# Attention of a three-stage kernel: turns in another order, mask and sums interleaved, weight transfers from ScalarE, mix's first key blocks around the last apply

## The chip, the cores and the metric

The kernel runs on one core of one Trainium2 chip. The metric is the device time of one execution in microseconds (us); lower is better. Engines are called by their names in the profile: PE is TensorE (PEld its weight loads), DVE is VectorE, ACT is ScalarE, POOL is GpSimd, SP is SyncE.

## The reference

Three stages follow each other: local and global attention, a gated channel mix, and a layer with eight experts of which each token takes one. The change lies in the first stage and in the first lines of the second.

```python
# attention: B=4, H=8 heads, 512 local and 32 global positions, head size 64
s_g  = scale * q_g @ concat(k_g, k_l).T              # global queries see all keys
out_g = softmax(s_g) @ concat(v_g, v_l)
s_ll = where(abs(i - j) <= 32, scale * q_l @ k_l.T, -1e9)
s_l  = concat(scale * q_l @ k_g.T, s_ll)             # local: a band, and the global keys
out_l = softmax(s_l) @ concat(v_g, v_l)              # softmax: exp(s - max) / (sum + 1e-9)
x = concat(out_g, out_l) as rows of 512, 2176 tokens in all
# mix
xk = mu_k * x + (1 - mu_k) * x_prev;  xr likewise with mu_r
x2 = sigmoid(xr @ w_r) * (relu(xk @ w_k) ** 2 @ w_v)
# experts: out = p[e] * (relu(x2 @ w1[e]) @ w2[e]), e chosen by token from its logits
```

## The kernel before

All is written by hand: each engine has its own program, the order on an engine is the order in the code, and semaphores tie the engines together.

Attention is cut into 40 units. A batch has ten (`UNITS`), in two quads (four heads each) of five: four local units of 128 queries by 160 keys for four heads, and one global unit (the 32 global queries against all 544 keys). A unit passes through these tasks:

- PE `scores` (L601 local, 16 matmuls; L615 global, 24) writes `ps_s`, which has two buffers.
- DVE `mask_scores` (L929, one instruction and the reading of its accumulator for each head; L933 for a global unit) writes `neg` and the negated maxima. `neg` has one buffer, so the mask of unit t starts after the exponentials of t-1.
- ACT `exponentials` (L1343, one for each head, with the row sums).
- POOL `copy_edges` (L456) gathers the columns of the global keys of four heads into `edge`, and POOL `spread_sums` (L466, L468) widens the inverted sums to `rb`. DVE `invert_sums` makes these (L942 adds 1e-9, L947 inverts).
- PE `turn` transposes: half a is two heads' probabilities (L630) and `rb` (L633), half b is the two other heads (L638) and `edge` (L640). `ps_t` has one buffer of two banks. ACT `copy_turned` (L1353) copies half a, DVE `copy_turned` (L955) half b, to `probT`.
- PE `apply` multiplies `probT` with the values (L668 with the global ones, L674 with the local ones; L686, L689, L692 in a global unit). It waits for both halves before its first matmul.
- DVE `write_x` (L966, L969) multiplies with the turned inverted sums into `xT`.

In step t PE does scores(t), apply(t-2), turn(t-1); DVE does invert(t-1), mask(t), write_x(t-2), copy(t-1); ACT does exponentials(t), copy(t-1). PE, DVE and ACT hold batches 1 and later in a loop; POOL is written out.

Between the units POOL prepares the mix's weights: 20 chunks of 128x512 arrive in two raw buffers (`w_raw`) by transfers that POOL issues itself (L433), POOL rounds a chunk (L437, `round_chunk`) and subtracts (L441, `rest_of_chunk`), then it issues the load of the chunk after next. Four such parts go to three steps, so the work ends with unit 29. In the last batch ACT and DVE also form the inputs of the mix's first group (`first_inputs`), with `w_raw`'s first half as scratch (`first_raw`); ACT therefore waits for all 20 chunks there. SP loads keys, queries and values (L349 to L360), each quad's for the next batch once its global unit has been scored or applied.

The mix takes four tiles of 128 tokens as a group. For each group PE forms eight blocks f of keys, each of 12 matmuls of 512 columns (L723 to L725: high by high, high by low, low by high), in two banks of PSUM in turn. Block f waits for the square of block f-2, which ACT (L1428) and DVE (L1063) make. Both begin the mix only when all of `xT` is written.

## Time and profile before

| | |
|---|---|
| median of 3 runs | 701.54 us (699.85 to 701.92) |
| the profiled execution, its own time | 700.96 us |
| its span | 699.3 us |
| busy over the span | PE 91%, DVE 52%, ACT 40%, POOL 26% |
| PE warms up (30 transposes) until | 7.1 us |
| first apply of attention starts | 13.45 us |
| PE busy from 150 to 300 us | 147.95 us |
| first matmul of the mix starts | 134.28 us |
| granted TensorE clock, mean | 0.966 (1.00 in every window up to 300 us) |

The span is the time between the first and the last instruction of the profiled execution; 1.7 us of that execution's time lie outside it. Times within the trace count from the span's start. A busy share over the whole span mixes the three stages. For this change the stretch from 7 to 140 us counts, and there the idle time of PE, with what ended it.

### The profile page before, as it was taken

What the parts mean: (1) busy time and instruction counts of PE and PEld (TensorE: products, weight loads), DVE (VectorE), ACT (ScalarE), POOL (GpSimd) and SP (SyncE); (2) the same over time, 40 slices, a digit from 0 to 9 for tenths busy, and PEclk for the clock granted to TensorE, in tenths of its full rate; (3) what the DMA queues carried; (4) which work ended last, traced back from release to release, by engine and by line L of the source; (5) the groups of instructions that cost most, each with busy time, mean ns of one, the idle gap of its engine ahead of it and who ended that gap; (6) DMA issues with size and microseconds to landing.
All of it is one profiled execution on the core that took longest, in us unless ns stands there. A gap on an engine that the chain in (4) does not pass through costs nothing.

```text
span 699.3 us, 15184 instructions
## 1 busy us (share of the span) xinstructions
PE 637.5 (91%) x4666; PEld 527.5 (75%) x4667; DVE 366.6 (52%) x920; ACT 281.6 (40%) x615; POOL 185.2 (26%) x263
## 2 busy tenths in 40 slices
PE   7899999899999999999999703999999999999994
PEld 6787777777887787789788502887888888888883
DVE  3677778594445626445434295649253353353531
ACT  4666678444313422332321140547243252262521
POOL 5676762200000000000000064235515215124140
PEclk9999999999999999999999855999999999999997
DMA  9878871000100010010010283658526135145000
GB/s 326 314 250 280 279 256 61 2 0 1 46 15 1 19 43 0 0 45 16 1 46 1 79 312 119 207 171 304 205 81 217 60 95 215 45 134 182 10 26 3
DMA packets 29204, 78.09 MB, mean 112 GB/s; under 512 B 4330, under 2 KB 7146, under 8 KB 29168
## 3 DMA queue, kind: packets, MB, share of 16 engines
q1 hardware_dynamic: 24368, 63.47, 26.1%
q0 software_dynamic: 4800, 14.16, 5.8%
q8 instruction: 19, 0.31, 0.2%
q14 instruction: 17, 0.14, 0.1%
HBM read 69.49 MB, written 9.70 MB: 113 GB/s over the span
## 4 chain that ended last, share of the span: by engine, by line
PE 81%; DVE 7%; ACT 5%; issue 4%; DMA 1%; POOL 0%; DVEq 0%; ACTq 0%; POOLq 0%
PE banks L723 22%; PE banks L725 21%; PE banks L724 21%; ACT prob L1343 3%; PE banks L869 3%; PE banks L742 2%; PE banks L668 1%; DMA xg<-x_rows,rows_in 1%; PE banks L844 1%; PE banks L630 1%; PE banks L615 1%; ACT probT L1353 1%; PE banks L674 1%; PE banks L734 1%; PE banks L686 1%
## 5 line engine op out<-in xcount | busy, mean ns | idle before, releaser
L518 POOL TENSOR_TENSOR we_lo<-we_raw,we_hi 128x1024 f32 (+1 forms) x18 | 50.4, 2822 | 319.8 <-ACT we_hi L1462 319.8
L1316 DVE TENSOR_SCALAR hid<-banks 128x512 f32<-128x512 f32 x40 | 27.7, 692 | 94.2 <-PE banks L725 92.8
L1343 ACT ACTIVATE prob<-neg,negmax 128x160 f32<-128x160 f32 (+1 forms) x136 | 59.2, 437 | 38.6 <-DVE negmax L929 27.4
L1462 ACT ACTIVATE we_hi<-we_raw 128x1024 f32 (+1 forms) x64 | 63.8, 1051 | 12.8 <-issue 8.1
L723 PE MATMUL banks<-we_hi,hid_hi 128*128 x160 | 66.8, 418 | 1.4 <-DVE hid_lo L1321 1.4
L723 PE MATMUL banks<-we_hi,xg_hi 128*128 x160 | 65.8, 411 | 1.7 <-DVE xg_lo L1287 1.7
L724 PE MATMUL banks<-we_lo,xg_hi 128*128 x160 | 63.8, 399 | 0.0
L725 PE MATMUL banks<-we_hi,xg_lo 128*128 x160 | 63.7, 398 | 0.0
L725 PE MATMUL banks<-we_hi,hid_lo 128*128 x160 | 63.1, 395 | 0.0
L724 PE MATMUL banks<-we_lo,hid_hi 128*128 x160 | 63.1, 394 | 0.0
L723 PE MATMUL banks<-mix_hi,wm_hi 128*128 128x512 f32 (+2 forms) x160 | 58.6, 366 | 0.5 <-DVE k_raw L1063 0.3
L725 PE MATMUL banks<-mix_hi,wm_lo 128*128 128x512 f32 (+2 forms) x160 | 57.2, 358 | 0.0
L724 PE MATMUL banks<-mix_lo,wm_hi 128*128 128x512 f32 (+2 forms) x160 | 57.1, 357 | 0.0
L1291 DVE TENSOR_TENSOR we_lo<-we_raw,we_hi 128x1024 f32 (+1 forms) x46 | 56.2, 1263 | 0.0
L723 PE MATMUL banks<-wm_hi,k_hi 128*128 128x512 f32 x136 | 54.0, 397 | 1.3 <-issue 1.3
L725 PE MATMUL banks<-wm_hi,k_lo 128*128 128x512 f32 x136 | 53.2, 391 | 0.0
L724 PE MATMUL banks<-wm_lo,k_hi 128*128 128x512 f32 x136 | 53.0, 390 | 0.0
L1495 ACT ACTIVATE hid_hi<-banks 128x512 fp32r<-128x512 f32 x40 | 23.9, 598 | 71.1 <-PE banks L869 71.1
L1428 ACT COPY k_sum<-banks 128x512 f32<-128x512 f32 (+2 forms) x40 | 20.9, 522 | 78.6 <-PE banks L725 78.5
L572 POOL DMA_INDIRECT out_rows<-y,rows_out x20 | 20.6, 1032 | 97.7 <-ACT y L1510 90.7
L1063 DVE SCALAR_TENSOR_TENSOR k_raw<-banks,k_sum 128x512 f32<-128x512 f32 (+2 forms) x40 | 24.4, 611 | 40.9 <-ACT k_sum L1428 40.9
L1321 DVE TENSOR_TENSOR hid_lo<-banks,hid_hi 128x512 fp32r<-128x512 f32 x40 | 27.6, 690 | 34.2 <-ACT hid_hi L1495 34.2
(215 smaller groups left out, 1400.6 us busy)
## 6 DMA issues: line engine op xcount, KB each, us to landing
we_raw<-in_w_e SPq DMA_DIRECT2D x64, 512.0 KB, 4.4
qk<-in_qk_t SPq DMA_DIRECT2D x32, 448.0 KB, 6.1
vw<-in_v_t SPq DMA_DIRECT2D x32, 256.0 KB, 4.5
w_raw<-in_w_mix POOLq DMA_DIRECT2D x20, 256.0 KB, 4.5
x_rows<-x SPq DMA_DIRECT2D x17, 256.0 KB, 2.0
vz<-in_v_z SPq DMA_DIRECT2D x8, 128.0 KB, 2.9
vx<-in_v_x SPq DMA_DIRECT2D x8, 96.0 KB, 5.1
qg<-in_qg_t SPq DMA_DIRECT2D x8, 64.0 KB, 6.8
```

Source lines behind the costliest of these rows:

```text
L518: return pool.tensor_tensor(we_lo[:, buf, 2 * j:2 * j + 2, :].rearrange("p x a b -> p x (a b)"), we_raw[:, j, :].unsqueeze(1), we_hi[:, bu ...
L723: pe.matmul(dst, left[0], right[0], start=first, stop=False)
L724: pe.matmul(dst, left[0], right[1], start=False, stop=False)
L725: return pe.matmul(dst, left[1], right[0], start=False, stop=last)
L869: mm = pe.transpose(ps_ht[:, h, P * c:P * (c + 1)], hid[:, D * h + P * c:D * h + P * (c + 1)], ident[:])
L1063: dve.scalar_tensor_tensor(raw, ps_k[:, f % 2, 0:w], 0.0, k_sum[:, f % 2, 0:w], ALU.max, ALU.mult).then_inc(k_squared, 1)
L1291: dve.tensor_tensor(we_lo[:, buf, 2 * j:2 * j + 2, :].rearrange("p x a b -> p x (a b)"), we_raw[:, j, :].unsqueeze(1), we_hi[:, buf, 2 * j ...
L1316: dve.tensor_scalar(hid[:, D * h:D * (h + 1)], ps_h[:, h, :], 0.0, None, ALU.max).then_inc(hid_ready, 1)
L1321: dve.tensor_tensor(hid_lo[:, D * h:D * (h + 1)], ps_ht[:, h, :], hid_hi[:, D * h:D * (h + 1)].bitcast(F32), ALU.subtract).then_inc(hid_lo ...
L1343: act.activation(prob[:, t % 2, c], neg[:, c], ACT.Exp, scale=-1.0, bias=negmax[:, t % 2, k:k + 1], accum_out=rsum[:, t % 2, k:k + 1]).the ...
L1462: act.activation(we_hi[:, buf, 2 * j:2 * j + 2, :].rearrange("p x a b -> p x (a b)"), we_raw[:, j, :].unsqueeze(1), ACT.Copy).then_inc(we_ ...
L1495: act.activation(hid_hi[:, D * h:D * (h + 1)], ps_ht[:, h, :], ACT.Copy).then_inc(hid_hi_ready, 1)
```

## The change

- **Turns.** `turn` does half b first (two heads, then `edge`), then half a: two heads, and `rb` as the last. ACT's exponentials and POOL's `spread_sums` wait for half a of the turn two units back, where they waited for half b. `edge` has one buffer instead of two, so `copy_edges(t)` waits for half b of turn t-1.
- **Apply.** It waits for half b alone at first, does the four matmuls with the global values and pair 1, waits for half a, then does pair 0. A global unit does its chunks 2, 3, 4 first, then 0 and 1.
- **Mask and sums.** In a local unit the mask's first head comes first, then the addition to the sums (`guard_sums`), the second head, the inversion (`invert_sums`), and the other two heads.
- **Weights.** ACT issues the 20 transfers: two at its start, then one after each `copy_turned` of an even step, behind a wait for POOL's subtraction. POOL rounds a chunk in an even step and subtracts it in the odd one, so the work ends with step 39. `first_raw` is a tile of its own, and ACT's wait for all chunks falls away. ACT's program is written out for all batches.
- **Mix.** Block 0 of group 0 is computed between the last turn and the last apply, behind a wait for all weight chunks; block 1 right after the last apply.

```diff
-        edge = sb("edge", [P, 2, HEADS * SG], to=att)
+        edge = sb("edge", [P, HEADS * SG], to=att)
...
-        first_raw = w_raw[:, 0, :]
+        first_raw = sb("first_raw", [P, GT * P], to=att)
...
-                if n + 2 < MIX_CHUNKS:
-                    pool.wait_ge(wm_lo_ready, n + 1)
-                    load_chunk(n + 2)
...
-                if n >= 2:
-                    pool.wait_ge(turned_b, n - 1)
+                if n >= 1:
+                    pool.wait_ge(turned_b, n)
                 by_head = prob[:, t % 2, :].rearrange("p (k c) -> p k c", k=HEADS)
-                pool.tensor_copy(edge[:, t % 2, :].rearrange("p (k c) -> p k c", k=HEADS),
-                                 by_head[:, :, HALO:KW]).then_inc(edged, 1)
+                pool.tensor_copy(edge[:].rearrange("p (k c) -> p k c", k=HEADS), by_head[:, :, HALO:KW]).then_inc(edged, 1)
...
-                    for part in range(4 * n // 3, 4 * (n + 1) // 3):
-                        if part >= 2 * MIX_CHUNKS:
-                            break
-                        if part % 2:
-                            rest_of_chunk(part // 2)
+                    n, low = divmod(UNITS * b + t, 2)
+                    if n < MIX_CHUNKS:
+                        if low:
+                            rest_of_chunk(n)
                         else:
-                            round_chunk(part // 2)
+                            round_chunk(n)
...
-                for k in range(2):
-                    c = KW * k if j is not None else P * k
-                    pe.transpose(ps_t[:, 0, P * k:P * (k + 1)], pr[:, c:c + P], ident[:])
-                pe.wait_ge(spread, n + 1)
-                for k in range(2 if j is not None else 1):
-                    mm = pe.transpose(ps_t[:, 0, P * (2 + k):P * (3 + k)], rb[:, t % 2, P * k:P * (k + 1)], ident[:])
-                mm.then_inc(turned_a, 1)
                 if j is not None:
                     for k in range(2):
                         c = KW * (2 + k)
                         pe.transpose(ps_t[:, 1, P * k:P * (k + 1)], pr[:, c:c + P], ident[:])
                     pe.wait_ge(edged, local_steps(b, t) + 1)
-                    mm = pe.transpose(ps_t[:, 1, 2 * P:3 * P], edge[:, t % 2, :], ident[:])
+                    mm = pe.transpose(ps_t[:, 1, 2 * P:3 * P], edge[:], ident[:])
                 else:
                     pe.transpose(ps_t[:, 1, 0:P], pr[:, 2 * P:3 * P], ident[:])
                     pe.transpose(ps_t[0:P - WIN, 1, P:2 * P], pr[:, 3 * P:SL - WIN], ident[:])
                     mm = pe.transpose(ps_t[0:WIN + SG, 1, 2 * P:3 * P], pr[:, SL - WIN:SL + SG], ident[:])
                 mm.then_inc(turned_b, 1)
+                for k in range(2):
+                    c = KW * k if j is not None else P * k
+                    pe.transpose(ps_t[:, 0, P * k:P * (k + 1)], pr[:, c:c + P], ident[:])
+                pe.wait_ge(spread, n + 1)
+                for k in range(2 if j is not None else 1):
+                    mm = pe.transpose(ps_t[:, 0, P * (2 + k):P * (3 + k)], rb[:, t % 2, P * k:P * (k + 1)], ident[:])
+                mm.then_inc(turned_a, 1)
...
-                pe.wait_ge(probT_a, n + 1)
...
                     for pair in range(2):
                         for h in range(2):
                             pe.matmul(o[DH * h:DH * (h + 1), P * pair:P * (pair + 1)], vz[i][:, 2 * pair + h, :],
-                                      pt(HEADS), start=True, stop=False)
+                                      pt(HEADS), start=(pair == 0), stop=False)
+                    for pair in (1, 0):
+                        if pair == 0:
+                            pe.wait_ge(probT_a, n + 1)
                         for blk in range(2):
                             for h in range(2):
                                 k = 2 * pair + h
                                 v0 = HEADS * DH * blk + DH * k
                                 mm = pe.matmul(o[DH * h:DH * (h + 1), P * pair + QB * blk:P * pair + QB * (blk + 1)],
-                                               vw[i][:, j, v0:v0 + DH], pt(k, QB * blk, QB), start=False, stop=(blk == 1))
+                                               vw[i][:, j, v0:v0 + DH], pt(k, QB * blk, QB), start=False, stop=(pair == 0 and blk == 1))
...
+                    for cs in ((2, 3, 4), (0, 1)):
+                        if cs[0] == 0:
+                            pe.wait_ge(probT_a, n + 1)
...
-            apply(B - 1, UNITS - 2)
-            turn(B - 1, UNITS - 1)
-            apply(B - 1, UNITS - 1)
...
+            def keys_part(g, tiles, f):
+                half, col = divmod(P * f, D)
+                for c in range(DC):
+                    mm = three_pass(ps_k[:, f % 2, 0:P * tiles], [a[:, HALVES * c + half, col:col + P] for a in wm],
+                                    [a[0][:, c, 0:P * tiles] for a in (mix_hi, mix_lo)], c == 0, c == DC - 1)
+                mm.then_inc(k_summed, 1)
+            apply(B - 1, UNITS - 2)
+            turn(B - 1, UNITS - 1)
+            pe.wait_ge(masked, heads_done(B - 1, UNITS - 1))
+            pe.wait_ge(mix_lo_ready, DC + 2)
+            pe.wait_ge(wm_lo_ready, MIX_CHUNKS)
+            keys_part(0, GT, 0)
+            apply(B - 1, UNITS - 1)
+            keys_part(0, GT, 1)
...
-                for f in range(FC):
+                for f in range(2 if first_group(g) else 0, FC):
...
+                        if last and k == 0:
+                            guard_sums(*last)
+                        if last and k == 1:
+                            invert_sums(*last)
...
-                if behind(b, t, 1):
-                    invert_sums(*behind(b, t, 1))
-                mask_scores(b, t)
+                last = behind(b, t, 1)
+                if last and unit(t)[1] is None:
+                    guard_sums(*last)
+                    invert_sums(*last)
+                mask_scores(b, t, last)
...
+            guard_sums(B - 1, UNITS - 1)
...
-                    act.wait_ge(turned_b, UNITS * b + t - 1)
+                    act.wait_ge(turned_a, UNITS * b + t - 1)
...
-                        act.wait_ge(wm_lo_ready, MIX_CHUNKS)
...
+            def load_chunk(n):
+                act.dma_start(w_raw[:, n % 2, :], w_mix[P * n:P * (n + 1), :]).then_inc(wm_raw_loaded[n % 2], 16)
...
+                n = (UNITS * b + t) // 2
+                if t % 2 == 0 and n >= 1 and n + 1 < MIX_CHUNKS:
+                    act.wait_ge(wm_lo_ready, n)
+                    load_chunk(n + 1)
+            for n in range(2):
+                load_chunk(n)
+            for b in range(B):
                 for t in range(UNITS):
                     step(b, t)
-            for t in range(UNITS):
-                step(B - 1, t)
-                first_inputs(t)
+                    if b == B - 1:
+                        first_inputs(t)
```

Three places show the new order. First PE in one local step of the first batch (apply of unit 1, turn of unit 2), before:

```order
L668 MATMUL banks<-probT,vz 64x128 [waits quad0_v1_loaded,probT_b,probT_a]
L668 MATMUL banks<-probT,vz 64x128
L674 MATMUL banks<-probT,vw 64x64 x4
L668 MATMUL banks<-probT,vz 64x128 x2
L674 MATMUL banks<-probT,vw 64x64 x4
L630 MATMUL banks<-ident,prob 128x128 [waits probT_b,probT_a,exped]
L630 MATMUL banks<-ident,prob 128x128
L633 MATMUL banks<-ident,rb 128x128 [waits spread]
L633 MATMUL banks<-ident,rb 128x128
L638 MATMUL banks<-ident,prob 128x128 x2
L640 MATMUL banks<-ident,edge 128x128 [waits edged]
```

and now (L657 and L666 are apply, L620 to L634 turn):

```order
L657 MATMUL banks<-probT,vz 64x128 [waits quad0_v1_loaded,probT_b]
L657 MATMUL banks<-probT,vz 64x128 x3
L666 MATMUL banks<-probT,vw 64x64 x4
L666 MATMUL banks<-probT,vw 64x64 [waits probT_a]
L666 MATMUL banks<-probT,vw 64x64 x3
L620 MATMUL banks<-ident,prob 128x128 [waits probT_b,probT_a,exped]
L620 MATMUL banks<-ident,prob 128x128
L622 MATMUL banks<-ident,edge 128x128 [waits edged]
L630 MATMUL banks<-ident,prob 128x128 x2
L634 MATMUL banks<-ident,rb 128x128 [waits spread]
L634 MATMUL banks<-ident,rb 128x128
```

The wait for `probT_a` moved from the first matmul of apply to the ninth, and the transposes of `rb` from the third and fourth place of the turn to the last.

Second, DVE in one local step, before (L942 and L947 are the sums of the unit before, L929 the mask with the reading of its accumulator, L969 write_x):

```order
L942 TENSOR_TENSOR rsum<-rsum,eps 128x4 [waits exped]
L947 RECIPROCAL rinv<-rsum 128x4 [waits spread,summed]
L929 ISA neg,negmax<-banks,mask 128x160 [waits scored,exped]
L929 ISA negmax 128x1
L929 ISA neg,negmax<-banks,mask 128x160
L929 ISA negmax 128x1
L929 ISA neg,negmax<-banks,mask 128x160
L929 ISA negmax 128x1
L929 ISA neg,negmax<-banks,mask 128x160
L929 ISA negmax 128x1
L969 TENSOR_TENSOR xT<-banks,probT 128x2x128 [waits applied]
L955 COPY probT<-banks 128x384 [waits applied,turned_b]
```

and now (L951 and L959 are the sums, L932 the mask):

```order
L932 ISA neg,negmax<-banks,mask 128x160 [waits scored,exped]
L932 ISA negmax 128x1
L951 TENSOR_TENSOR rsum<-rsum,eps 128x4 [waits exped]
L932 ISA neg,negmax<-banks,mask 128x160
L932 ISA negmax 128x1
L959 RECIPROCAL rinv<-rsum 128x4 [waits spread,summed]
L932 ISA neg,negmax<-banks,mask 128x160
L932 ISA negmax 128x1
L932 ISA neg,negmax<-banks,mask 128x160
L932 ISA negmax 128x1
L981 TENSOR_TENSOR xT<-banks,probT 128x2x128 [waits applied]
L967 COPY probT<-banks 128x384 [waits applied,turned_b]
```

The mask's first head no longer stands behind the sums; the inversion stands behind two heads of the mask.

Third, ACT at the end of steps 1 and 2, before:

```order
L1353 COPY probT<-banks 128x512 [waits turned_a]
L1343 ACTIVATE prob,rsum<-neg,negmax 128x160 [waits masked,turned_b]
L1343 ACTIVATE prob,rsum<-neg,negmax 128x160 [waits masked] x3
L1353 COPY probT<-banks 128x512 [waits turned_a]
L1343 ACTIVATE prob,rsum<-neg,negmax 128x160 [waits masked,turned_b]
```

and now (L1358 is an exponential, L1368 the copy, L1388 a weight transfer):

```order
L1368 COPY probT<-banks 128x512 [waits turned_a]
L1358 ACTIVATE prob,rsum<-neg,negmax 128x160 [waits masked,turned_a]
L1358 ACTIVATE prob,rsum<-neg,negmax 128x160 [waits masked] x3
L1368 COPY probT<-banks 128x512 [waits turned_a]
L1388 DMA w_raw<-in_w_mix 128x512 [waits wm_lo_ready]
L1358 ACTIVATE prob,rsum<-neg,negmax 128x160 [waits masked,turned_a]
```

The transfer waits for POOL's subtraction, and the exponentials of the next step are queued behind it.

Last, PE at the end of attention, before (turn of unit 39 from `rb` on, its apply, the mix):

```order
L633 MATMUL banks<-ident,rb 128x128 [waits spread]
L642 MATMUL banks<-ident,prob 128x128
L643 MATMUL banks<-ident,prob 96x128
L644 MATMUL banks<-ident,prob 64x128
L686 MATMUL banks<-probT,vw 64x32 [waits x_written,quad1_vx_loaded,probT_b,probT_a]
L686 MATMUL banks<-probT,vw 64x32 x5
L689 MATMUL banks<-probT,vw 64x32 x2
L692 MATMUL banks<-probT,vx 64x32 x2
L686 MATMUL banks<-probT,vw 64x32 x6
L689 MATMUL banks<-probT,vw 64x32 x2
L692 MATMUL banks<-probT,vx 64x32 x2
L723 MATMUL banks<-mix_hi,wm_hi 128x512 [waits mix_lo_ready,k_squared,wm_lo_ready,consts_loaded]
```

and now:

```order
L630 MATMUL banks<-ident,prob 128x128 x2
L634 MATMUL banks<-ident,rb 128x128 [waits spread]
L714 MATMUL banks<-mix_hi,wm_hi 128x512 [waits wm_lo_ready,mix_lo_ready,masked]
L715 MATMUL banks<-mix_lo,wm_hi 128x512
...
L716 MATMUL banks<-mix_hi,wm_lo 128x512
L681 MATMUL banks<-probT,vw 64x32 [waits quad1_vx_loaded,x_written,probT_b]
L681 MATMUL banks<-probT,vw 64x32
L685 MATMUL banks<-probT,vw 64x32 x2
...
L688 MATMUL banks<-probT,vx 64x32 x2
L681 MATMUL banks<-probT,vw 64x32 [waits probT_a]
L681 MATMUL banks<-probT,vw 64x32 x7
L714 MATMUL banks<-mix_hi,wm_hi 128x512
L715 MATMUL banks<-mix_lo,wm_hi 128x512
```

Twelve matmuls of the mix stand between the turn and the apply.

## Rows read from the trace of the kernel before

**Rows 1.** Windows of one quad each: bounds; span, busy time (instructions) by engine; clock; DMA.

```profile
24.96:41.72 16.76, 14.56 (x259) 12.01 (x259) 11.25 (x55) 10.21 (x39) 11.31 (x22) 1.00 0.79 260
...
86.72:101.70 14.98, 14.15 (x258) 11.86 (x259) 11.28 (x56) 10.45 (x40) 10.81 (x19) 1.00 0.78 279
101.70:117.67 15.97, 14.15 (x258) 11.85 (x258) 13.96 (x59) 13.25 (x45) 3.31 (x9) 1.00 0.32 103
117.67:132.71 15.04, 12.91 (x227) 10.91 (x227) 11.80 (x49) 10.30 (x34) 4.68 (x24) 1.00 0.00 1
```

**Rows 2.** Chain of waits, 82 to 93 us: start, length, engine, what, line.

```profile
86.72 0.54 PE banks L686 x12
...
88.08 0.37 PE banks L630 x2
...
89.61 0.18 DVE rsum L942
...
90.10 0.33 DVE neg L929
...
92.22 0.48 ACT probT L1353
...
92.75 0.32 PE banks L668
```

**Rows 3.** Timeline of one local step: start, length, engine, line, [idle before, releaser].

```profile
89.81 0.18 DVE L947 RECIPROCAL rinv<-rsum 128x4 f32<-128x4 f32 x1
...
90.06 0.40 POOL L468 COPY rb<-rinv 128x256 f32<-128x256 f32 x1 [0.59 <-DVE rinv L947]
...
91.66 0.77 PE L601 MATMUL banks<-qk 64*64 64x160 f32 x15
...
92.74 0.33 DVE L929 CUSTOM_DVE_ANT_0 neg<-banks,mask 128x160 f32<-128x160 f32 x1
...
92.99 0.32 DVE L929 CUSTOM_DVE_ANT_0 neg<-banks,mask 128x160 f32<-128x160 f32 x1
...
93.11 0.43 ACT L1343 ACTIVATE prob<-neg,negmax 128x160 f32<-128x160 f32 x1 [0.41 <-DVE negmax L929]
...
93.80 0.44 PE L630 MATMUL banks<-ident,prob 128*128 128x128 f32 x2
...
94.71 1.30 PE L615 MATMUL banks<-qk,qg 128*64 128x128 f32 x24
...
96.22 0.72 DVE L933 TENSOR_SCALAR_CACHE_REDUCE neg<-banks 128x544 f32<-128x544 f32 x1 [0.56 <-PE banks L615]
```

**Rows 4.** SyncE issues of line 358: engine, operation, nanoseconds min/median/max, first and last.

```profile
L358 SPq DMA_DIRECT2D vw<-in_v_t x32: 427/436/1406, 3.7 to 104.9; - x32
```

**Rows 5.** The tile w_raw until 125 us: GpSimd instructions, landing, waiters.

```profile
L433 POOL DMA_DIRECT2D w_raw<-in_w_mix x20: 559/559/730, 4.6 to 92.7; - x20
...
L441 POOL TENSOR_TENSOR wm_lo<-w_raw,wm_hi x20: 1265/1272/1277, 13.8 to 99.7; 128x512 fp32r<-128x512 f32 x20
...
  POOL wm_hi L437: 5.3, 3
...
DMA to landing us min/median/max: 2.9/4.5/7.0
```

**Rows 6.** Timeline of TensorE, the first apply and a stall in step 7.

```profile
13.45 0.44 PE L668 MATMUL banks<-probT,vz 128*64 128x128 f32 x4 [0.68 <-ACT probT L1353]
...
29.24 0.49 PE L601 MATMUL banks<-qk 64*64 64x160 f32 x3 [1.32 <-issue]
```

**Rows 7.** Timeline at the end of attention, GpSimd and TensorE.

```profile
130.31 0.29 POOL L466 COPY rb<-rinv 128x128 f32<-128x128 f32 x1 [1.99 <-DVE rinv L947]
...
131.73 0.27 PE L644 MATMUL banks<-ident,prob 128*64 128x128 f32 x1
...
132.71 0.54 PE L686 MATMUL banks<-probT,vw 128*64 128x32 f32 x12 [0.70 <-ACT probT L1353]
...
134.28 0.47 PE L723 MATMUL banks<-mix_hi,wm_hi 128*128 128x512 f32 x1 [0.22 <-DVEq L1015]
```

92 lines of the change are left out of this document (42 added, 50 removed).

## The prediction

> **What bounds the kernel now.** I first cut attention into quads, from the apply of one global unit to that of the next [rows 1]. Between 41.72 and 101.70 us lie four quads, 59.98 us, so 15.0 us each, or 3.00 us a step. PE is busy for 14.15 us of such a quad; with its 258 or 259 matmuls that is a floor of 2.83 us a step. The quad before lasts 16.76 us (14.56 busy), the two of the last batch 15.97 and 15.04. PE is therefore the engine nearest to its limit, and what it loses is small: 0.8 us in a common quad.
>
> The chain of waits says who takes that [rows 2]. A loop over two steps goes from apply to apply: 88.08-86.72 = 1.36 for the apply of a global unit; 89.61-88.08 = 1.53 for the turn, DVE's copy and the start of the sums; 0.49 for the sums; 92.22-90.10 = 2.12 from the mask's first head over four exponentials to ACT's copy; 0.53 for that copy. The sum is 6.03 us, 3.01 a step, where PE alone would need less. The timeline shows the same from PE's side: the mask starts at 92.74, 0.3 us after the scores end (91.66+0.77), since the sums stand ahead of it, and the apply starts at 92.75, behind the copy [rows 2, 3]. From 150 to 300 us PE is busy for 147.95 us (the table above), so what is won before the mix should reach the end whole.
>
> **The change part by part.** *Apply on half a unit, half b turned first.* The apply now waits for DVE's half alone; ACT's half is needed for its last third, roughly. The apply of a local unit takes 93.80-92.75 = 1.05 us, so the loop holds 0.35 instead of 1.05 to 1.36 of it. *The mask's first head ahead of the sums.* The new path from the turn to the mask runs through the scores: 94.71-93.80 = 0.91 for the turn, 0.77 for the scores, 96.22-(94.71+1.30) = 0.21 until DVE starts, 1.89 together, against 2.02 over the sums [rows 2, 3]. The two small instructions come between the heads: a head is due every 92.99-92.74 = 0.25 us, an exponential 0.43 us, so pushing the second and third head back by 0.16 to 0.2 us delays the exponentials by 0.1 us at most. New loop: 0.35+1.89+2.12+0.1+0.53 = 4.99 us in two steps, 2.5 a step. That is under the floor of 2.83, so this loop no longer binds.
>
> *What is late next.* `rb` is now turned last, but its sums are also made later. From the mask's start: head 0.25, addition 0.16, head 0.25, inversion 0.18, 90.06-(89.81+0.18) = 0.07 to POOL, 0.40 for `rb`, 0.05 back to PE, in all 1.36 us; with two waits on registers in the loops I allow up to 1.5 (the hand-overs but the first are estimates by that 0.07). Then come two transposes (0.22), the gap to the scores (0.14), the scores (0.77) and 0.21 until the next mask: 2.70 to 2.84 us a step [rows 3]. This second loop lies beside PE's floor of 2.83, and in a local step behind a local apply, whose own floor is about 2.73, it costs up to 0.1 us. I count three such steps in a quad, 0.3 us: a quad of 14.15+0.3 = 14.45 us. The bounds are 14.15 (nothing waits) and 15.0 (all comes back in the second loop; that needs 0.2 us more in each local step than I allow).
>
> *Mid quads:* four times 15.0-14.45 = 0.55, 2.2 us. *First quad after the start:* of its 16.76 us, 1.32 are a stall of PE in the middle of one unit's scores, which waits for no semaphore [rows 6]; I leave it in, so 15.44 comes down to about 14.5, 0.9 us (bounds 0.4 and 2.3). *Start:* PE idles 0.68 us before its first apply, behind ACT's copy [rows 6]; half b is there earlier, the mask of the second unit starts sooner, but the first turn waits longer for `rb`. I take half, 0.35 us.
>
> *Last batch.* PE needs 14.15 and 12.91 us there, and DVE is busy for 13.96 of 15.97 us [rows 1]: with the mix's inputs DVE has a loop of its own near 15.97/5 = 3.2 us a step. The turn's half b first removes DVE's wait for the turn, the sums no longer hold the mask back, but ACT now also issues four transfers there. I take 0.5 us in each of the two quads (bounds -0.5 and 1.2): 1.0 us.
>
> *Block 0 of the mix before the last apply.* PE idles 0.70 us for ACT's copy before the last apply and 0.22 us before the mix [rows 7]. Twelve matmuls of 512 columns cover both. The price is the wait for the last chunk: POOL now subtracts it after the last `rb`, 130.31+0.29+1.27 = 131.87 by the old clock, and the last turn ends at 131.73+0.27 = 132.00 [rows 5, 7]. So the wait is 0 to 0.3 us, and I count 0.92-0.17 = 0.75 us. Block 1 needs no square; block 2 does, and both squares are made within the 2.8 us of block 1, as ACT and DVE may begin right after the last write of `xT`.
>
> *Weights from ACT.* POOL loses 20 issues of 0.56 us, which cost nothing before except where POOL was late. Its own waits for chunks, 5.3 us in three [rows 5], lay behind loads landing 2.9 to 7.0 us after their issue; now a chunk is issued some 6 us ahead of its rounding, so I expect few. ACT pays: in a step of 2.83 us it has four exponentials (2.12-(93.11-92.74) = 1.75 at most) and a copy (0.53), which leaves 0.55 us [rows 2, 3]. An issue is not shown on ACT; the nearest rows are SP's, 0.43 to 1.41 us with a median of 0.44, and POOL's 0.56 [rows 4, 5]. At 0.44 it fits. It also waits for POOL's subtraction: mask start + 1.3 (`rb` written) + 1.27 = 2.6, against 2.12+0.53 = 2.65 when ACT is through its copy. That too fits, narrowly. I cost it at nothing; the cover is ACT's 0.55 us, and what is over it delays the next exponentials, and PE from about 0.4 us further on. At 1.41 us it would be 0.4 us or so in each of 18. The two first transfers, 0.5 MB, now start ahead of SP's first tiles instead of behind them. PE's warm-up, 30 transposes until 7.1 us (the table above), hides them.
>
> The Trainium skill, Perfetto Trace Analysis, under DMA Instruction for HWDGE, says that the descriptor hardware is locked for one issuer at a time and that the time of an issue includes the wait for that lock. This trace agrees as far as it goes: SP's issues differ by three times [rows 4], but nothing here shows two issuers. By the rule an issue of ACT that meets one of SP takes up to 0.9 us instead of 0.44; SP makes eleven issues in a quad, 4.8 us of some 14.5, so 6 of 18 would, each 0.35 us over the cover, 2.1 us in all, and the time would be 698.4.
>
> **The sum.** 2.2+0.9+0.35+1.0+0.75 = 5.2 us. The profiled execution took 700.96 us (span 699.3, 1.7 outside it) and would take 695.8. The median of the runs is 701.54, 0.58 above it; by that I predict 696.3 us.
>
> **Rivals.** *The second loop takes the place of the first.* If the sums reach PE 0.2 us later than I allow, quads stay at 15.0. For it: the path has six handovers between four engines, and the registers of the loops add to some. Against it: each handover shown takes under 0.1 us. Then only start (0.35), tail (0.75), part of the last batch (0.5) and of the first quad (0.4) remain, 2.0 us: 699.5. Chance 0.2.
>
> *Slower: ACT's transfers.* Place: ACT between copy and the next exponentials, 18 times. If wait and issue together take 1.2 us, half a microsecond comes over the cover and what PE can bear; 18 times 0.5 = 9 us against a gain of 5.2: 705.3. It breaks even at 0.9 us per transfer. For it: SP's longest issues, and POOL's subtraction ending just as ACT wants to go on. Against it: SP's median of 0.44. Chance 0.13.
>
> *The floor.* If nothing waits, quads take 14.15 us: 3.4 in the four, 2.0 in the first quad with part of the stall gone, 0.5, 1.7 and 0.9: 8.5 us, 693.0. For it: in most windows PE's busy time is the same to 0.01 us. Against it: the second loop. Chance 0.12.
>
> *The change does not reach the end.* The mix could give back what attention won, if DVE, which squares its first blocks, sets the pace there. The idle time of PE there is under 1 us, so this is the smallest, 698 or so: 0.05.
>
> **How the numbers follow.** The forecast, 696.3 with its own range of 694.5 to 698.5, has 0.5. A measurement of this kernel tells about 0.3% from no change, 2.1 us, so faster means under 699.4. The forecast, the floor and the last rival are faster (0.67), and of the second-loop case a little, 0.05: 0.72. Its rest, and a mild form of ACT's, are the same: 0.18. Slower: 0.10. The range for 8 in 10 goes from 693.0, the floor, to 700.5, which leaves out the worse part of ACT's case and of the second loop.
>
> **What would show it.** Right: quads of 14.3 to 14.6 us with PE busy for 14.15; PE's waits for ACT's `probT` gone; small waits for `rb` in turn; ACT's issues near 0.44 us; 12 matmuls of the mix between the last turn and the last apply with under 0.3 us of idle time before them. Wrong: quads of 15 us with waits for `rb` (second loop), ACT idle before its transfers or transfers of 0.9 us and more (ACT's case), waits of POOL for chunks, or a first scores task after 7.3 us. A stall like the one at 29.24 us elsewhere would move the time by 1.3 us without any of this.

## The result and the profile after

| | before | after |
|---|---|---|
| median of the runs | 701.34 us (699.85 to 701.92, 4 runs) | 689.39 us (689.20 to 689.47, 4 runs) |
| ratio, 95% interval | | 0.983 [0.982, 0.985] |
| profiled execution, its span | 700.96, 699.3 us | 689.36, 687.5 us |
| start of the first 128x32 matmul of an apply, first and last (global units) | 24.96, 132.71 | 24.01, 124.15 |
| start of the mix's third key block | 139.84 | 128.29 |

The change is 12 us faster; 5.2 were forecast, and the time lies below the range. The last line tells where: 11.55 us of it are won by the start of the third key block, up to which both kernels do the same work. What follows, which no kernel below changes, took 559.5 us before (699.3-139.84), 559.2 after and 557.1 to 560.5 in the others, so a total carries some 1.5 us either way that have nothing to do with attention. Starts in the trace are therefore used beside the totals; the granted clock is 1.00 in both traces from 7 to 300 us.

The windows of one quad each, cut at the apply of a global unit as in [rows 1] (bounds; span, busy time and instructions of each engine, granted clock, DMA share, GB/s):

```profile
24.01:37.98 13.97, 13.95 (x262) 11.83 (x259) 10.26 (x55) 10.33 (x40) 7.76 (x14) 1.00 0.86 299
...
79.94:94.07 14.13, 14.05 (x262) 11.85 (x259) 10.31 (x55) 10.55 (x41) 7.70 (x14) 1.00 0.78 267
94.07:108.16 14.09, 14.09 (x259) 11.81 (x259) 13.45 (x60) 12.95 (x45) 7.64 (x15) 1.00 0.61 203
108.16:124.15 15.99, 15.54 (x242) 13.03 (x239) 12.03 (x51) 10.57 (x35) 10.73 (x30) 1.00 0.05 17
```

A quad takes 14.0 instead of 15.0 us, and PE is busy for nearly all of it (13.95 to 14.09 us), in the last batch too. The last window holds a key block of the mix (124.15-121.22 = 2.93 us) and would be 13.06 without it.

The chain of waits over two steps (start, length, what, line) shows the same. Where [rows 2] went through ACT's copy, the sums and the mask, it stays on PE:

```profile
83.97 0.37 PE banks L620 x2
84.34 0.11 PE banks L622
84.45 0.22 PE banks L630 x2
84.67 0.27 PE banks L634 x2
84.93 0.70 PE banks L590 x16
85.64 0.59 PE banks L657 x8
86.22 0.47 PE banks L666 x16
86.69 0.37 PE banks L620 x2
```

One local step on the timeline, against [rows 3] (start, length, engine, line):

```profile
83.80 0.17 DVE L959 RECIPROCAL rinv<-rsum 128x4 f32<-128x4 f32 x1
...
84.04 0.40 POOL L461 COPY rb<-rinv 128x256 f32<-128x256 f32 x1 [1.04 <-DVE rinv L959]
...
84.50 0.43 PE L634 MATMUL banks<-ident,rb 128*128 128x128 f32 x2
...
84.86 0.77 PE L590 MATMUL banks<-qk 64*64 64x160 f32 x16
...
85.57 0.66 PE L657 MATMUL banks<-probT,vz 128*64 128x128 f32 x8
...
85.95 0.32 DVE L932 CUSTOM_DVE_ANT_0 neg<-banks,mask 128x160 f32<-128x160 f32 x1 [0.71 <-PE banks L590]
...
86.75 0.40 POOL L461 COPY rb<-rinv 128x256 f32<-128x256 f32 x1 [0.98 <-DVE rinv L959]
...
87.22 0.42 PE L634 MATMUL banks<-ident,rb 128*128 128x128 f32 x2
```

PE waits for nobody in this step, but `rb` is just in time: it is written at 84.44 and 87.15, and turned 0.06 and 0.07 us later. This is the second loop of the prediction, and its period can be added up: 84.86-84.50 = 0.36, 85.95-84.86 = 1.09, 86.75-85.95 = 0.80, 87.22-86.75 = 0.47, together 2.72 us, the length of the step.

The other rows: the tile `w_raw`, against [rows 5] (nanoseconds min/median/max, first and last start), and the waiter for the last chunk, against [rows 7]:

```profile
L1388 ACTq DMA_DIRECT2D w_raw<-in_w_mix x20: 334/334/462, 0.9 to 111.0; - x20
L434 POOL CAST wm_hi<-w_raw x20: 612/614/617, 11.8 to 117.8; 128x512 fp32r<-128x512 f32 x20
L438 POOL TENSOR_TENSOR wm_lo<-w_raw,wm_hi x20: 1268/1272/1277, 14.5 to 119.8; 128x512 fp32r<-128x512 f32 x20
...
  PE banks L714: 0.2, 1
...
DMA to landing us min/median/max: 2.5/4.6/7.3
```

An issue takes ACT 0.334 us, 0.46 at most; POOL no longer waits for a chunk. The first apply starts at 13.04 us, 0.41 earlier than before [rows 6], and the stall of 1.32 us in the first quad [rows 6] is gone. Where an issue lies between its neighbours (POOL's subtraction, ACT's copy, the issue, the next exponential):

```profile
25.50 1.28 POOL L438 TENSOR_TENSOR wm_lo<-w_raw,wm_hi 128x512 fp32r<-128x512 f32 x1
...
26.77 0.56 ACT L1368 COPY probT<-banks 128x512 f32<-128x512 f32 x1
26.81 0.34 ACTq L1388 DMA_DIRECT2D w_raw<-in_w_mix  x1
27.68 0.43 ACT L1358 ACTIVATE prob<-neg,negmax 128x160 f32<-128x160 f32 x1 [0.35 <-DVE negmax L932]
```

The issue does wait for the subtraction: 15 of the 18 in the steps start 0.03 us after it ends. But it runs beside ACT's copy, not behind it, and ends 0.28 to 1.17 us before the next exponential.

### The profile page after: what moved, and what is told of

Same layout as the page of the kernel before. It is cut to its first block, busy times and chain, and to the rows that moved or that the text cites. A ratio compares the mean times of both kernels' runs of the same rounds, so it can differ in the third digit from the quotient of the medians.

```text
span 687.5 us, 15076 instructions
## 1 busy us (share of the span) xinstructions
PE 636.6 (93%) x4666; PEld 527.9 (77%) x4667; DVE 359.1 (52%) x920; ACT 281.6 (41%) x615; POOL 174.8 (25%) x243
## 4 chain that ended last, share of the span: by engine, by line
PE 88%; DVE 7%; issue 2%; DMA 1%; ACT 1%; POOL 1%; DVEq 0%; ACTq 0%; POOLq 0%
PE banks L714 22%; PE banks L716 22%; PE banks L715 21%; PE banks L590 3%; PE banks L873 3%; PE banks L657 2%; PE banks L750 2%; PE banks L666 2%; PE banks L620 1%; DMA xg<-x_rows,rows_in 1%; PE banks L848 1%; PE banks L604 1%; PE banks L742 1%; PE banks L634 1%; PE banks L630 1%
## 5 line engine op out<-in xcount | busy, mean ns | idle before, releaser
L1358 ACT ACTIVATE prob<-neg,negmax 128x160 f32<-128x160 f32 (+1 forms) x136 | 59.1, 436 | 29.3 <-DVE negmax L932 19.6
L932 DVE CUSTOM_DVE_ANT_0 neg<-banks,mask 128x160 f32<-128x160 f32 x128 | 37.7, 315 | 25.7 <-PE banks L590 24.5
```

The lines of the kernel that those rows point to most:

```text
L932: dve.tensor_tensor_reduce(neg[:, KW * k:KW * (k + 1)], s[:, h, KW * pair:KW * (pair + 1)], mask[:, m, :], -SCALE, HUGE, ALU.add, ALU.min, ...
L1358: act.activation(prob[:, t % 2, c], neg[:, c], ACT.Exp, scale=-1.0, bias=negmax[:, t % 2, k:k + 1], accum_out=rsum[:, t % 2, k:k + 1]).the ...
```

## The experiments

Each ratio is to the kernel before (its medians were 701.1, 701.2, 700.9 and 700.8 in the four sets of experiments). "u" kernels are the changed kernel with one part undone. The last two columns are from the profiled run: the start of the mix's third key block, and the time to it from the first apply of a global unit, where the first quad begins.

| kernel | median us | ratio [95%] | quads (first; four mid, mean) | third key block | from the first quad on |
|---|---|---|---|---|---|
| before | 701.3 | 1 | 16.76; 15.00 | 139.8 | 114.9 |
| after | 689.4 | 0.983 [0.982, 0.985] | 13.97; 14.02 | 128.3 | 104.3 |
| u_order | 700.1 | 1.000 [0.998, 1.002] | 15.25; 15.23 | 139.8 | 113.7 |
| u_turn | 698.6 | 0.995 [0.994, 0.997] | 15.06; 15.06 | 138.9 | 112.6 |
| u_apply | 694.9 | 0.991 [0.989, 0.993] | 14.99; 14.91 | 135.5 | 110.1 |
| u_weights | 696.7 | 0.994 [0.992, 0.996] | 16.04; 14.89 | 134.3 | 109.2 |
| u_pool2 | 690.5 | 0.984 [0.982, 0.986] | 13.97; 14.05 | 128.8 | 104.4 |
| u_plan43 | 690.7 | 0.987 [0.983, 0.990] | 14.68; 14.14 | 129.9 | 104.9 |
| u_mask | 689.6 | 0.985 [0.982, 0.988] | 13.88; 13.89 | 127.9 | 104.0 |
| u_mix | 689.0 | 0.984 [0.981, 0.986] | 13.97; 14.02 | 129.5 | 104.3 |
| sums_late | 701.1 | 1.000 [0.999, 1.002] | 15.51; 15.63 | 141.5 | 115.2 |
| minimal | 692.3 | 0.986 [0.982, 0.990] | 14.76; 14.25 | 131.9 | 106.6 |
| o_order | 694.3 | 0.991 [0.989, 0.994] | 16.00; 14.74 | 133.5 | 109.8 |
| o_weights | 699.1 | 0.997 [0.995, 0.998] | 15.11; 15.03 | 139.2 | 113.4 |
| o_even | 701.3 | 1.001 [1.000, 1.003] | 15.11; 15.10 | 138.8 | 113.9 |
| o_unroll | 701.4 | 1.001 [0.999, 1.003] | 15.98; 15.01 | 139.4 | 114.4 |

The start of a trace has a disturbance of its own. In six of the sixteen profiled executions (u_order, u_turn, u_apply, u_weights, u_plan43, u_mix) the granted clock is 0.50, the lower of its two levels (1.2 GHz), for 3.4 us that begin between 11.4 and 12.9 us; before it PE had stood for 1.97 us, waiting for the first exponentials, as it does in the changed kernel and before, where the clock stays at 1.00. In u_mix the step that starts at 11.98 takes 4.21 us so, where the changed kernel takes 2.67 (12.33 to 15.00). That is 1.5 us, and the quads, which begin later, are free of it; the last column therefore compares better than the one before it. How many of the other runs behind a median had it is not known.

The times of u_order, u_apply, u_mix, o_order and o_weights fell in none of the ranges expected of them, and u_turn's lies between two of its own. o_unroll's first quad (15.98 us) fell in neither of its two ranges.

**The order on PE.** u_order takes it back whole: half a and the sums turned first, and both waits ahead of the apply. u_turn takes back the turn alone, u_apply the split wait alone (with the turn, POOL and ACT wait for half b again, as before):

```diff
 def turn(b, t):                      # u_order, u_turn
+    (half a, pe.wait_ge(spread, n + 1), rb)
     (half b)
-    (half a, pe.wait_ge(spread, n + 1), rb)
...
 def apply(b, t):                     # u_order, u_apply
+    pe.wait_ge(probT_a, n + 1)
     pe.wait_ge(probT_b, n + 1)
```

Expected of u_order:

> The changed kernel with the order on TensorE undone: half a turned first, apply waits for both halves before its first matmul (edge keeps its one buffer). Theory L (the two-step loop over ACT's copy and the whole apply was the brake, and the order opened it): the loop closes again at 1.05 to 1.36 + 1.89 + 2.2 + 0.53, about 5.8 us in two steps, quads of 14.5 to 14.8 us, 695 to 697 us in all. Theory W (the weights on POOL were the brake, by their late chunks and by the stall of 1.3 us): little is lost, 690 to 691 us.

Expected of u_turn:

> The changed kernel with half a and the sums turned first, as before, and the split wait of the apply kept (half b's blocks first, half a's wait behind them). Theory L: rb is again wanted early in the turn, and half b is turned last, so ACT's copy is due at the start of the apply, where half b is used first: the loop over ACT's copy and a whole apply is back, 699 to 701, quads of 15.2, waits of PE for probT written by ACT. Theory S (the split wait alone counts): 690 to 693. With both terms partly right, 695 to 698.

Expected of u_apply (it names the copies the wrong way round: DVE copies half b, ACT half a, so it is ACT's copy that the last turned half waits for):

> The changed kernel in which the apply waits for both copied halves before its first matmul, as before; the turn keeps its new order (half b, then half a and the sums). After took 689.4, and the same kernel with the old turn as well took 700.1. In the new order ACT's half b is copied first and DVE's half a last, so at the apply only DVE's copy can be late. Theory L (the two-step loop that ran over ACT's copy and the whole apply): turning half b first already takes ACT's copy off the loop, and DVE's copy of half a is short, but the apply's first two thirds no longer cover it: 0.2 to 0.4 us of idle PE before each of 34 applies unless the scores stand between, 691 to 694, quads of 14.1 to 14.5. Theory S (only the split wait counts, since it gives the copies time): 697 to 700, quads of 15. If the turn's order is all: 689 to 690.

Without the new order no gain clear of noise is left (1.000, 0.998 to 1.002). The waits of u_order from 13 to 121 us (engine, line, releaser: us in total, times, longest):

```profile
PEld banks L658 <- ACT probT L1369: 3.9, 13, 0.5
...
PEld banks L623 <- POOL rb L461: 3.3, 11, 0.3
PEld banks L682 <- ACT probT L1369: 2.4, 4, 0.8
```

and of u_apply:

```profile
PEld banks L658 <- ACT probT L1369: 6.6, 17, 0.7
...
PE banks L682 <- ACT probT L1369: 2.8, 7, 0.4
```

So the loop over ACT's copy and a whole apply is what held 3.0 us a step, as the prediction read it from the chain. (u_order's mid quads are 0.23 us longer still than before: its sums stand within the mask, and PE waits 3.3 us for `rb`, where it waited 0.5 before.) The turn is worth 9.2 us on top of the split wait (698.6-689.4), the split wait 5.5 on top of the turn (694.9-689.4), both 10.7; by the traces from the first quad on 8.3, 5.9 and 9.4. In u_apply the mid quads are still 14.91 us: against the 15.00 before, turning half b first gains little there while the apply waits for both halves. (Against u_order it gains 5.2 us; by the trace from the first quad on 3.6, of which 1.3 lie in the four mid quads and 2.0 in the last batch.) In u_turn PE waits for `rb` and for DVE's copy of half b (4.8 and 4.1 us) instead of ACT's.

**The weights.** u_weights gives the transfers back to POOL, with the old plan of four half-roundings in three steps:

```diff
+                if n + 2 < MIX_CHUNKS:
+                    pool.wait_ge(wm_lo_ready, n + 1)
+                    load_chunk(n + 2)
...
-                    n, low = divmod(UNITS * b + t, 2)
...
+                    for part in range(4 * n // 3, 4 * (n + 1) // 3):
...
-                    act.wait_ge(wm_lo_ready, n)
-                    load_chunk(n + 1)
```

> The changed kernel with the weight transfers back on POOL and its old plan, four parts in three steps (ACT stays written out, first_raw stays a tile of its own). Theory L: POOL has room, so 690 to 691 us. Theory W: the waits of POOL for chunks and the stall in the scores come back, and rb, now turned last, is late behind them: 693 to 697 us, with waits of PE for rb.

It costs 7.3 us, where my prediction had the weights at nothing; by the trace from the first quad on it is 5.0. PE waits for `edge`, not for `rb` as expected. Its waits from 13 to 121 us, and POOL around the longest of PE:

```profile
POOL wm_hi L437 <- DMA w_raw<-in_w_mix: 6.6, 6, 2.2
POOL w_raw L433 <- POOL wm_lo L441: 5.3, 18, 0.3
PEld banks L632 <- POOL edge L456: 5.1, 8, 1.5
...
PE banks L632 <- POOL edge L456: 2.9, 5, 1.3
```

```profile
28.08 0.62 POOL L437 CAST wm_hi<-w_raw 128x512 fp32r<-128x512 f32 x1 [1.47 <-DMA w_raw<-in_w_mix]
...
28.79 1.27 POOL L441 TENSOR_TENSOR wm_lo<-w_raw,wm_hi 128x512 fp32r<-128x512 f32 x1
...
30.35 0.56 POOL L433 DMA_DIRECT2D w_raw<-in_w_mix  x1 [0.30 <-POOL wm_lo L441]
30.91 0.30 POOL L456 COPY edge<-prob 128x128 f32<-128x128 f32 x1
...
31.14 0.41 POOL L467 COPY rb<-rinv 128x256 f32<-128x256 f32 x1
```

`edge` is made at 30.91, behind a subtraction, a wait of 0.30 us and an issue of 0.56, and PE, which could turn it 1.30 us before, stands until 31.27. Two kernels part the two halves of this. u_pool2 has the issues on POOL and the even plan; u_plan43 has the issues on ACT and the crowded plan (ACT's at its pace):

```diff
-                if t % 2 == 0 and n >= 1 and n + 1 < MIX_CHUNKS:      # u_plan43
-                    act.wait_ge(wm_lo_ready, n)
-                    load_chunk(n + 1)
+                m = UNITS * b + t
+                for n in range(1, MIX_CHUNKS - 1):
+                    if m == (3 * n + 1) // 2:
+                        act.wait_ge(wm_lo_ready, n)
+                        load_chunk(n + 1)
```

> The changed kernel with the weights issued by GpSimd again, but with the changed kernel's even plan (one half of a chunk's rounding a step) in place of four parts in three steps. With both of the old things it took 696.7, with neither 689.4. Theory W1 (the issues and the waits for the transfer behind them cost: a 0.56 us issue, 0.3 us of wait ahead of it, and a load that lands after it is wanted): about 694 to 697, GpSimd still waits 5 us or more for chunks. Theory W2 (the crowding costs: in each third step GpSimd has 1.9 us of rounding between two edges, with the issue 2.8): the even plan gives most back, 690 to 692, PE's waits for edge under 0.5 us in all.

> The changed kernel (weights from ScalarE) with the old uneven plan of GpSimd, four parts in three steps, ScalarE's transfers following it at that pace. W1 (the issues cost): 689 to 691. W2 (the crowding costs): 692 to 696, with waits of PE for edge or rb of about 3 us. If the gain of the weights is one of both together, this one and the one with GpSimd's issues in the even plan are each within 1.5 us of 689.4.

Each costs about 1 us, both together 7.3; by the trace from the first quad on 0.1, 0.6 and 5.0. (u_plan43's four runs lie between 688.9 and 694.0, so its 1 us is the least certain.) The rows above say why. In the fullest step POOL has `edge` and `rb` (0.30+0.41), and then with the crowded plan both parts of a chunk (0.61+1.27) and the issue with its wait (0.56+0.30): 3.45 us, more than a step of 2.8. With the issue moved away it is 2.59; with the even plan, whose fullest step has the subtraction and the issue, 2.84. Either edit alone brings POOL to about the length of a step. This account is worked out, not tested by itself, and it leaves out the chunk's landing: ahead of the longest wait POOL also stood 1.47 us for a transfer, though not ahead of the four other waits of PE for `edge` (0.30 to 0.52 us). Late chunks alone are not enough: in u_plan43 POOL waits 8.0 us for them, more than the 6.6 here, and little is lost.

**The sums.** u_mask has the sums ahead of the whole mask, as before; sums_late has the inversion behind the fourth head instead of the second:

```diff
-                if last and unit(t)[1] is None:          # u_mask
+                if last:
                     guard_sums(*last)
...
-                        if last and k == 1:              # sums_late
+                        if last and k == 3:
                             invert_sums(*last)
```

> The changed kernel with the sums again ahead of the whole mask. Theory L: the sums stand behind DVE's copy, which comes early when half b is turned first, so the mask starts hardly later: 689.5 to 691 us. Theory M (the early first head is a main part): the mask is 0.3 us late in each step, 40 steps, 694 us or more.

> The changed kernel with the inversion of the row sums behind the fourth head of the mask instead of the second, which makes rb about 0.5 us later in every step. It probes the slack of the second loop (sums, GpSimd's rb, its transposes, scores, mask), on which the prediction counted 0.1 us a step and its rival all of the gain. If that loop has under 0.1 us of slack, each of some 36 steps loses 0.3 to 0.5 us: 700 to 705. With a slack of 0.3 us: 692 to 696. With over 0.5 us (the copies of half b and the apply cover it): 689 to 690, no waits of PE for rb.

u_mask: the interleave gains nothing. In the trace it even costs 0.14 us a mid quad (14.02 against 13.89), since with the sums first `rb` is ready early and a local step as the one above is 2.67 us, PE's own length:

```profile
84.96 0.66 PE L657 MATMUL banks<-probT,vz 128*64 128x128 f32 x8
85.03 0.18 DVE L959 RECIPROCAL rinv<-rsum 128x4 f32<-128x4 f32 x1
85.27 0.40 POOL L461 COPY rb<-rinv 128x256 f32<-128x256 f32 x1
...
86.62 0.38 PE L634 MATMUL banks<-ident,rb 128*128 128x128 f32 x2
```

sums_late: the second loop is real and at its limit. Making `rb` 0.5 us later gives back all 12 us (two of its ten runs took 1631.9 and 825.9 us, which nothing here explains). A quad grows by 15.63-14.02 = 1.6 us; of its five steps two take the half microsecond whole, two take 0.3 and 0.4 us of it, and one hides it. A step that waits:

```profile
92.28 0.32 DVE L932 CUSTOM_DVE_ANT_0 neg<-banks,mask 128x160 f32<-128x160 f32 x1 [1.03 <-PE banks L590]
...
93.34 0.17 DVE L959 RECIPROCAL rinv<-rsum 128x4 f32<-128x4 f32 x1
...
93.58 0.40 POOL L461 COPY rb<-rinv 128x256 f32<-128x256 f32 x1 [1.34 <-DVE rinv L959]
...
94.03 0.44 PE L634 MATMUL banks<-ident,rb 128*128 128x128 f32 x2 [0.31 <-POOL rb L461]
```

**The mix block.** u_mix puts both key blocks behind the last apply:

```diff
-            keys_part(0, GT, 0)
             apply(B - 1, UNITS - 1)
+            keys_part(0, GT, 0)
             keys_part(0, GT, 1)
```

> The changed kernel with both key blocks after the last apply. By all theories the idle time before the last apply comes back: 0.7 to 0.9 us, 690.1 to 690.3 us. If the block before the apply also hid DVE's and ACT's start of the mix, up to 1.5 us.

From the apply of the next to last global unit to the third key block it takes 129.49-109.34 = 20.15 us, the changed kernel 128.29-108.16 = 20.13, the kernel before 139.84-117.67 = 22.17. The placement is worth nothing, where 0.7 to 0.9 us were expected; the 2.04 us there come with the order.

**One part alone.** o_order is the kernel before with the new order on PE alone; o_weights has the weights from ACT and the even plan alone; o_even the even plan alone; o_unroll ACT's attention loop written out alone. minimal has two edits, order and even plan, with the issues left on POOL. The shared lines are those of the diffs above; o_unroll's:

```diff
-            with act.Fori(1, B - 1) as b:
+            for b in range(B):
                 for t in range(UNITS):
                     step(b, t)
```

> The kernel before with the new order on PE alone (turn b first, split apply, sums turned last, one edge buffer); weights still issued by GpSimd in the old plan, sums whole ahead of the mask, mix's blocks after the last apply. After without the move of the weights took 696.7. Theory W (GpSimd's weight waits make edge late, worth 7 us once the order is in): 696 to 698, with GpSimd's waits for the chunks about 12 us and PE's waits for edge 2 to 3 us. Theory L alone (order is all, the 7 us of that run came from something else): 690 to 692.

> The kernel before with the weights issued by ScalarE (its attention loop written out), GpSimd's two-step plan and one edge buffer; order of PE, sums and mix as before. Theory L (ScalarE's copy and the whole apply hold the loop at 3.0 us a step): GpSimd is not on that loop, so 700 to 701.5, quads of 15.0. Theory W (GpSimd's lateness is a brake of its own): 694 to 696. The 1.32 us stall inside one unit's scores in the first quad: if GpSimd's issues or the loads made it, it is gone and the first quad takes 15.4; if it is code loading of one engine, it stays or moves.

> The kernel before with the even plan alone (and the scratch of the mix's inputs in its own tile, one edge buffer); order on PE, issues by GpSimd, sums and mix as before. If the loop over ScalarE's copy and the whole apply holds the step: 699 to 701, mid quads of 15.0, first quad 15.1 to 15.4 if the crowded plan made the stall of 1.32 us, 16.8 if the issues by GpSimd did. If GpSimd's crowding was a brake of its own: 695 to 697.

> The kernel before with ScalarE's attention loop written out and nothing else. The 1.32 us stall of PE in the first quad was gone in every kernel with ScalarE's loop written out. If the loop's entry on ScalarE made it, the first quad takes 15.3 to 15.5 instead of 16.76 and the time is 699.7 to 700.3; if the transfers issued by GpSimd or their landing made it, 16.5 to 16.8 and 701.2. The mid quads stay at 15.0 in both.

> The kernel before with two edits only: the new order on PE (half b turned and applied first, sums turned last) and GpSimd's even plan of one part a step. Weights still issued by GpSimd, sums whole ahead of the mask, the mix's blocks after the last apply. If order and plan carry all: 688.5 to 690.5, quads of 13.9. If moving the issues, the sums or the mix block matter beyond them: 691 to 694.

(o_order, o_even and minimal have ACT's loop written out too and the mix's inputs in a tile of their own; o_unroll shows that the first is worth nothing.) o_weights gains 2 us, and the 15.0 us of the mid quads stay: the weights do not touch the old loop. In its trace 1.5 us lie between the first quad's start and the third key block, all of it in the first quad (15.11 us), where the stall of 1.32 is missing; o_even has the same 15.11 and gains nothing in its median, so what the 2 us come from is open. o_order gains 7; its mid quads lie between 13.88 and 15.39 us. The parts alone make 7 and 2, all together 12. o_order's median is 2.4 us below that of u_weights, which has the interleave and the early mix block as well, but the intervals meet, and from the first quad on u_weights is 0.5 us the shorter.

minimal settles at 13.88 us a quad, as u_mask, but carries stalls of PE that wait for no semaphore, of the kind of the 1.32 us before [rows 6]:

```profile
21.89 0.27 PE L642 MATMUL banks<-ident,rb 128*128 128x128 f32 x1 [0.70 <-issue]
28.87 0.35 PE L598 MATMUL banks<-qk 64*64 64x160 f32 x1 [0.54 <-issue]
43.58 0.27 PE L642 MATMUL banks<-ident,rb 128*128 128x128 f32 x1 [1.30 <-issue]
```

One of its four runs took 689.1, the others 692.3 to 693.6. Its 692.3 lies in the second range expected, 691 to 694, but not for the reason given there: without the stalls (2.54 us in the profiled run) it would be at about 690, an estimate, and so in the first.

**The stalls without a semaphore.** From 13 to 121 us o_order has three of 0.4 us or more (0.56, 0.74, 0.85), minimal three, o_unroll one (0.48) and the kernel before one (1.32); the other twelve have none. The traces say what they are. They list DMA packets of 16 KB of the kind "instruction", eight of them by 67 us and then none until the mix, so they come while PE runs through its code for the first time and not when its loop repeats it. Each of the eight stalls ends 1.35 to 1.63 us after such a packet has ended (the one at 29.24 after a packet from 26.59 to 27.64 us), and each of these packets came late, counted by the matmuls and weight loads that PE had begun when it started: at its place in the order of packets, none that no such stall follows starts as late in any of the sixteen traces. The second packet, for one, starts at 639 to 672 in the kernel before, minimal, o_order and o_unroll, at 635 in u_weights (a stall of 0.21 us), and at 493 to 559 in the eleven others. So PE waited for its own code, as far as traces can tell; no run delays a packet on purpose.

**What stays open.** What makes a packet late. All five kernels with a late second packet issue the weights from POOL, and four of them have the crowded plan, yet u_pool2 and o_even issue from POOL too and have it early; ACT's written-out loop neither makes nor removes the stalls. With one profile of each kernel, chance is not excluded.

## Why the prediction was wrong

The direction, the loop that holds the kernel and PE as the next bound were right. Sizes were wrong, and every term was too small: the step that failed is the pricing, above all of the quads (the floor of 14.15 us, the stall left in, DVE's loop in the last batch). By the steps of the sum, each measured between the same marks of the two traces:

| term | forecast | measured |
|---|---|---|
| start, to 24.96 and 24.01 | 0.35 | 0.95 |
| first quad, 16.76 and 13.97 | 0.9 | 2.8 |
| four mid quads, 59.98 and 56.09 | 2.2 | 3.9 |
| first quad of the last batch, 15.97 and 14.09 | 0.5 | 1.9 |
| rest to the third key block, 22.17 and 20.13 | 0.5+0.75 | 2.0 |
| sum | 5.2 | 11.55 |

*Mid quads.* "A quad of 14.15+0.3 = 14.45 us" failed at both terms. The floor of 14.15 was PE's busy time in a trace in which PE waited; the last matmul before a wait counts to its end, while without a wait the next one starts before that end (the scores are 0.77 us long, and the apply now starts 85.57-84.86 = 0.71 us after their start). The same instructions are busy for 14.76 us a quad in sums_late and for 13.88 in u_mask, where no wait is left; and of the four mid quads before, one had 14.66, not 14.15:

```profile
56.48:71.84 15.36, 14.66 (x258) 11.86 (x259) 11.72 (x55) 10.31 (x39) 10.59 (x20) 1.00 0.82 279
```

And the second loop was allowed 2.70 to 2.84 us and counted 0.3 us a quad; it is 2.72, 0.05 above PE's 2.67 in such a local step, and the interleave costs 0.14 us a quad against u_mask.

*First quad.* "I leave it in" was wrong: the stall of 1.32 us went, and the order took 1.5 of the rest. Whether the change removed the stall or a run happens to be free of it isn't settled: the late code packet behind it came early in the changed kernel (at 22.80 us, 540 matmuls and weight loads), and why is open.

*Start.* Half of the 0.68 us was taken; 0.95 came. In the traces at full clock the kernels with the new order (the 0.70 us stall of minimal taken off) have their first global apply at 23.7 to 24.7 us, those with the old one at 24.9 to 25.8, sums_late apart, so the sign holds and the size is good to half a microsecond.

*Last batch.* DVE was read as having "a loop of its own near 3.2 us a step" there. It had not: with 13.45 us of work it fits into 14.09. The 13.96 busy in 15.97 was high use in a loop that others held. This is the largest relative miss: 1.0 forecast, 1.9 and most of 2.0 measured.

*Mix block.* 0.75 us for covering 0.92 of idle time. Half of the idle time left by itself when the order changed: u_mix idles 0.48 us before the last apply and not at all before the mix. The block covers that, but waits 0.23 us for the last chunk itself, and u_mix is at the same 20.15 us.

*Weights from ACT.* They were costed "at nothing" against the old profile, and o_weights bears that out but for 2 us that nothing here places. The error was to stop there. What the changed order needs was not asked: in the quicker steps POOL's 3.45 us no longer fit, and without the move and the even plan 7.3 of the 12 us do not come. That does not lower the forecast, which assumed the move; it shows how the forecast came to rest on a part that had no term.

ACT's side held for another reason than the one given: the 0.55 us behind the copy were hardly needed, since each of the 18 issues starts before the copy has ended, by 0.17 to 0.58 us. The wait for the subtraction is real, in 15 of 18 steps, and "fits, narrowly" was right: 0.28 us is the least that was left.

*The rivals.* ACT's transfers: an issue took 0.334 to 0.362 us in the steps, and no exponential waited for it. The price of the rival was also out of line with the prediction's own cover: with 0.55 us for ACT and 0.4 more for PE, 1.2 us leave 0.25, not 0.5, so 4.5 us instead of 9, 700.8 instead of 705.3, and break even at 1.24 us instead of 0.9. By the Trainium skill, Perfetto Trace Analysis, DMA Instruction — HWDGE, an issue's time includes the wait for the lock, and this trace agrees, but the wait it leaves room for is small. Twelve issues that met none of SP's took 0.334 or 0.335 us. Six of the eighteen in the steps met one, as many as reckoned, and took 0.334 to 0.362; the two at the start took 0.409 and 0.462. The estimate of 0.9 us was far off, and 698.4 with it. The second loop: wrong as a forecast of this kernel, right as a mechanism, since sums_late shows that half a microsecond more in it costs the whole gain. The floor was the nearest, 693.0, and even it was 3.6 us too high: by the table above 0.5 us in the four mid quads, 0.8 in the first, 0.45 at the start and 1.3 in the last batch with the tail.

## What to carry to other kernels

Busy time of a pipelined engine in a loop that another engine holds is no floor: it grows with the waits, and the true one is seen only where nothing waits (here 13.88 us a quad, against 14.15 to 14.76 for the same instructions). When two changes each shorten a loop whose next limits lie close together, price them together: order and weights gave 7 and 2 alone and 12 together (with two parts that are worth nothing), and undoing the two halves of the weights' part cost about 1 us each but 7 together. And sum an engine's work in its fullest step, not its mean (3.45 us against a step of 2.8).

## What the hardware showed unasked

Issuing a 256 KB transfer took 0.334 us on ACT and ran beside ACT's copy, where the same transfer took 0.559 on POOL and needed a wait of 0.30 for its own last write; SP's were 0.43 us. PE can stand for 0.5 to 1.3 us in the first 50 us with no semaphore to wait for, 1.35 to 1.63 us behind a late 16 KB packet of instructions, in some kernels and not in their near twins, and this came to 2.5 us in minimal's profiled run. And the granted clock fell to 1.2 GHz for 3.4 us near 12 us in six of sixteen executions, which cost 1.5 us where it could be compared.
